# Row sums turned before the reciprocal instead of after it, in the attention stage of an attention and MLP kernel

## The chip, the cores and the metric

The kernel runs on one core of a Trainium2 chip. The metric is the device time in microseconds of one execution. Before the change it is 834.61 us, the median of 3 runs (834.24 to 835.53).

## The reference: attention, then two MLPs

Attention over 4 x 8 heads of 576 rows with 64 elements, with a decay bias from cumulative sums, and on its output (2304 tokens x 512) two MLPs. What the change touches is the division of the softmax by its sum:

```python
scores = np.where(causal, -1000000000.0, scores + np.minimum(bias, 0.0))
scores = scores - np.max(scores, axis=-1, keepdims=True)
attn = np.exp(scores)
attn = attn / (np.sum(attn, axis=-1, keepdims=True) + 1e-09)
return np.matmul(attn, v).astype(np.float32)
```

The first MLP computes (h - tanh(h)) @ w_out with h = x @ w_in (512 to 2048 to 512), the second a softmax-weighted, normalised hidden layer (512 to 1024 to 512). Their code is not touched.

## The kernel before, in words

Heads are worked in 16 pairs. A head's 576 rows are four tiles of 128 and a tail of 64; the tails of a pair's two heads share one tile, so a pair has 9 tiles (`TILES`). The attention stage is a software pipeline of slots, numbered -1 to 17: slot s loads and turns q and k of pair s+1, scores and exponentiates pair s, turns the probabilities of pair s-1 and multiplies them by V, and ends and scales pair s-2. Slots -1 to 3 and 14 to 17 are written out; slots 4 to 13 are a hardware loop of two slots a turn. "Slot 11" below is the one in which pair 11 is scored. In slots 16 and 17 no scores are left, and the first tiles of the first MLP's first chunk stand between the attention's matmuls.

There is no scheduler. Each engine has its own instruction list in the order of the code, and semaphores are the only ties between them; a wait stops everything behind it on its engine.

What each engine does for a slot:

- TensorE: `score` (three float32r products a tile, a mask matmul last), `turn_p` (transposes of the probabilities into PSUM, units A01, A2, A3, T, B01, B2, B3), `turn_qk` (transposes of q and k), `attend` (probabilities times V: `attend(-2, 1, ...)` ends the second head of pair s-2, `attend(-1, 0, ...)` does the first head of pair s-1) and, once a pair, the turn of the 9 columns with the softmax denominators (L1354 to L1360).
- VectorE: `bias` (L1000, adds the cumulative bias to the scores, PSUM to SBUF, and finds the row's extreme), `p_lo` (L983, the low part of the turned probabilities: PSUM minus the rounded high part), `x_add` and `x_low_part` (L1023, L1014, sums of the attend product), and `denominators` (L1025 to L1033).
- ACT: `p_hi` (L737, rounds the turned probabilities to the high part), `exp` (L746, with the row sum accumulated into a column of `row_sum`), `qk_copy` (L763), `x_low_part(0)` (L778), `rden_rows_copy` (L765 to L771).
- POOL: `sums` (L539, L542, copies the tail of the cumulative sums), `split_qk` (L557, L560), `scale_x` (L579, multiplies by the spread reciprocals), `split_v` (L592, L595).
- SP: the loads, the store of `rden_row` to HBM (L444, L446) and its broadcast back (L462).

The denominators of a pair are 9 columns of 128 values, one column a tile. VectorE adds 1e-9 (L1031) and takes the reciprocal (L1033) of the whole 128 x 9 array in SBUF; TensorE turns it into 9 rows of 128 in PSUM (L1360), ACT copies the rows to SBUF (L771), and SP stores them so that they can be read back broadcast over 64 partitions for `scale_x` in the next slot.

TensorE's first `attend(-1, 0, 0)` of a slot waits for `p_lo("T")`, which VectorE issues after `bias(0, 0)`, `bias(0, 1)`, `x_add(0)`, `p_lo("A01")`, `bias(1, 0)`, `bias(1, 1)`, `denominators()`, `p_lo("A2")`, `bias(0, 2)`, `bias(1, 2)`, `p_lo("A3")`, `x_low_part(1)` and `x_add(1)`. TensorE's `score(3)` waits for `bias(0, 2)`, whose PSUM it writes over.

Of the kernel before, what the change touches and what calls it, by code (L numbers as in the profile page):

```python
# [6 lines left out]
ALU = mybir.AluOpType  # L7
# [7 lines left out]
P = 128  # L15
# [35 lines left out]
def build_transformer(nc, q, k, v, s, w_in, w_out, w2_in, w2_out, g_ln, out):  # L51
# [59 lines left out]
    with ctx:  # L111
# [12 lines left out]
        with ExitStack() as phase:  # L124
            sb = tensors(phase, attention_words)
            qkT_hi = [sb(f"qkT_hi{n}", [P, QK_W], F32R) for n in range(2)]
            qkT_lo = [sb(f"qkT_lo{n}", [P, QK_W], F32R) for n in range(2)]
            probs = [sb(f"probs{n}", [P, PW]) for n in range(2)]
            pT_hi = sb("pT_hi", [P, 2, PT_W], F32R)

            v_parts = [sb(f"v_parts{n}", [P, NT, 4 * D], F32R) for n in range(2)]
            ident_b = sb("ident_b", [P, P], BF16)
            mask_b = sb("mask_b", [P, P], BF16)
            upper_b = sb("upper_b", [P, TAIL], BF16)
            lower_b = sb("lower_b", [P, TAIL], BF16)
            tail_mask_b = sb("tail_mask_b", [P, TAIL], BF16)
            neg_max = [sb(f"neg_max{n}", [P, TILES]) for n in range(2)]
            row_sum = [sb(f"row_sum{n}", [P, TILES]) for n in range(2)]
            den = [sb(f"den{n}", [P, TILES]) for n in range(2)]
            rden = [sb(f"rden{n}", [P, TILES]) for n in range(2)]  # L140
            rden_row = sb("rden_row", [TILES, P])

            w1i_words = GATE_W + FT * 2 * DM
            sb("gap", [P, w1i_words - sum(attention_words)])
            cum_bc = [sb(f"cum_bc{n}", [P, 2, S]) for n in range(2)]
            cum_tail = sb("cum_tail", [P, S])
            v_raw = [sb(f"v_raw{n}", [P, NT, 2 * D]) for n in range(2)]
            pT_lo = sb("pT_lo", [P, 2, PT_W], F32R)
            rden_T = [sb(f"rden_T{n}", [P, S]) for n in range(2)]
            qk_flat = [sb(f"qk_flat{n}", [P, FULL * P]) for n in range(2)]  # L150
            x_low = sb("x_low", [P, S])
            x_sum = sb("x_sum", [P, S])
# [64 lines left out]
        turn_ps = {"A01": bank(3), "A2": bank(4), "A3": bank(3), "T": bank(4), "B01": bank(3), "B2": bank(5), "B3": bank(4)}  # L217
        qk_ps = bank(5)

        rden_ps = bank(6)[0:TILES, 0:P]  # L220
        x_ps = psum[:, 7 * BANK - X_CUT:7 * BANK - X_CUT + S]
        h_ps = [bank(n, CH) for n in (0, 1, 2, 3)]
        y_ps = [bank(m, CH) for m in (4, 5, 6, 7)]
# [31 lines left out]
        biased = sem("biased")  # L255
        exped = sem("exped")
        den_step = sem("den_step")
        turned_rden = sem("turned_rden")
        rden_rows = sem("rden_rows")
        turned_p = sem("turned_p")  # L260
        p_hi_done = sem("p_hi_done")
# [407 lines left out]
        def _(act):  # L669
# [60 lines left out]
            def slot(sl):  # L730
                def p_hi(unit):

                    if sl.runs(-1):
                        pair, half, par = sl.pair(-1)
                        act.wait_ge(turned_p, UNITS * pair + NTH[unit])
                        for ps, to in pieces(unit):
                            hi = act.activation(to(pT_hi), ps, ACT.Copy)  # L737
                        hi.then_inc(p_hi_done, 1)

                def exp(h, t):  # L740

                    if sl.runs(0):
                        pair, half, par = sl.pair(0)
                        at, width, col = tile_at(h, t)
                        act.wait_ge(biased, TILES * pair + nth(sl, h, t)[0])
                        act.activation(probs[par][:, at:at + width], probs[par][:, at:at + width], ACT.Exp,  # L746
                                       bias=neg_max[par][:, col:col + 1], scale=-1.0,
                                       accum_out=row_sum[par][:, col:col + 1]).then_inc(exped, 1)

                def qk_copy(n):  # L750

                    if sl.runs(1):
                        pair, half, par = sl.pair(1)
                        at, width = QK_PART[n]
                        act.wait_ge(turned_qk, 3 * pair + n + 1)

                        if sl.fixed and sl.s <= 0:
                            to = qkT_hi[par][:, at:at + width]
                        else:
                            to = qk_flat[n % 2][:, 0:width]  # L760
                            if n != 1:
                                act.wait_ge(qk_lo, 3 * pair + (n == 2))
                        act.activation(to, qk_bank(sl, n)[:, 0:width], ACT.Copy).then_inc(qk_copied, 1)  # L763

                def rden_rows_copy():  # L765

                    if sl.runs(-1):
                        pair, half, par = sl.pair(-1)
                        act.wait_ge(turned_rden, pair + 1)
                        wait(act, rden_out, 32 * pair)  # L770
                        act.activation(rden_row[:, :], rden_ps, ACT.Copy).then_inc(rden_rows, 1)  # L771

                def x_low_part(h):

                    if sl.runs(-2):
                        pair, half, par = sl.pair(-2)
                        act.wait_ge(attended, 2 * pair + h + 1)
                        act.activation(x_low[h * D:(h + 1) * D, :], x_ps[(1 - h) * D:(2 - h) * D, :],  # L778
                                       ACT.Copy).then_inc(x_low_done, 1)

                if sl.fixed and sl.s == 0:
                    for h in range(2):
                        exp(h, 0)
                        exp(h, 1)
                    qk_copy(0)
                    exp(0, 2)
                    qk_copy(1)
                    exp(1, 2)
                    qk_copy(2)
                    exp(0, 3)  # L790
                    exp(1, 3)
                    exp(None, FULL)
                    return
                x_low_part(0)
                p_hi("A01")
                exp(0, 0)
                p_hi("A2")
                qk_copy(0)
                exp(0, 1)
                exp(1, 0)  # L800
                exp(1, 1)
                first_w1i(sl, 0)
                p_hi("A3")
                qk_copy(1)
                rden_rows_copy()
                exp(0, 2)
                if sl.fixed and sl.s == LAST:

                    act.wait_ge(turned_p, UNITS * PAIRS)
                    act.wait_ge(v_split, 2 * PAIRS)  # L810
                    step(0, 0)
                p_hi("T")
                first_w1i(sl, 1)
                qk_copy(2)
                exp(1, 2)
                p_hi("B01")
                exp(0, 3)
                first_w1i(sl, 2)
                p_hi("B2")
                exp(1, 3)  # L820
                first_w1i(sl, 3)
                p_hi("B3")
                exp(None, FULL)
# [82 lines left out]
        def _(dve):  # L906
# [69 lines left out]
            def slot(sl):  # L976
# [29 lines left out]
                def x_low_part(h):  # L1006

                    if sl.runs(-2):
                        pair, half, par = sl.pair(-2)
                        dve.wait_ge(attended, 2 * pair + h + 1)  # L1010
                        if h == 1 and sl.runs(-1):

                            dve.wait_ge(rden_rows, pair + 2)
                        dve.tensor_copy(x_low[h * D:(h + 1) * D, :], x_ps[(1 - h) * D:(2 - h) * D, :]).then_inc(x_low_done, 1)  # L1014

                def x_add(h):
# [8 lines left out]
                def denominators():  # L1025

                    if sl.runs(-1):
                        pair, half, par = sl.pair(-1)
                        dve.wait_ge(exped, TILES * (pair + 1))
                        wait(dve, turned_rden, pair - 1)  # L1030
                        dve.tensor_scalar(den[par][:, :], row_sum[par][:, :], 1e-9, None, ALU.add).then_inc(den_step, 1)  # L1031
                        dve.wait_ge(den_step, 2 * pair + 1)
                        dve.reciprocal(rden[par][:, :], den[par][:, :]).then_inc(den_step, 1)  # L1033

                def qk_rest(n):

# [28 lines left out]
                p_lo("A01")  # L1065
                bias(1, 0)
                bias(1, 1)
                denominators()
                p_lo("A2")
                bias(0, 2)  # L1070
                bias(1, 2)
                first_w1i(sl, 0)
# [110 lines left out]
        def _(pe):  # L1183
# [58 lines left out]
            def slot(sl):  # L1242
# [108 lines left out]
                            mm = pe.transpose(to[:, TAIL:TAIL + P], q_raw[par][:, FULL, :], ident[:, :])  # L1351
                        mm.then_inc(turned_qk, 1)

                def turn_rden():  # L1354

                    if sl.runs(-1):
                        pair, half, par = sl.pair(-1)
                        pe.wait_ge(den_step, 2 * (pair + 1))
                        wait(pe, rden_rows, pair)
                        pe.transpose(rden_ps, rden[par][:, :], ident[:, :]).then_inc(turned_rden, 1)  # L1360

                if sl.fixed and sl.s == 0:
                    score(0, 1)
# [10 lines left out]
                turn_qk(0)  # L1374
                score(2)
                attend(-2, 1, 0)
                turn_p("A3")
                turn_qk(1)
                turn_rden()
                attend(-2, 1, 1, 2, 3, 4)  # L1380
                turn_p("T")
                turn_qk(2)
# [109 lines left out]
```

## Time and profile before

| | |
|---|---|
| median of 3 runs | 834.61 us |
| profiled execution, in all | 835.15 us |
| its span | 833.3 us |
| TensorE matmuls busy | 816.6 us, 98% |
| VectorE busy | 446.4 us, 54% |
| ACT busy | 384.7 us, 46% |
| POOL busy | 200.2 us, 24% |
| mean granted TensorE clock | 0.996 |

```profile
## 2 busy tenths in 40 slices
PE   6999999998999999999999999999999999999998
DVE  5789999998854332233223322334647554455442
ACT  4899899888543322223223222324524333333322
POOL 3687787788100000000000000000022211221110
PEclk9899999999999999999999999999999999999999
```

PE is TensorE, DVE is VectorE. Each digit is the busy share of a fortieth of the span, 20.8 us, in tenths. The attention stage is the first ten or eleven slices: there VectorE and ACT are as busy as TensorE, and POOL nearly so; behind it TensorE is alone. A matmul's end is modelled, so a busy TensorE is not one at its peak. In the rows, times are microseconds unless marked ns; in brackets stands the idle time of an engine before an instruction and what ended it.

### The profile page before, as it was taken

The page shows a single profiled execution, that of the slowest core. Times are in us where ns is not written, and L with a number is a line of the kernel's source. Part 1 is how long each engine was busy: PE and PEld are TensorE (multiplying, and loading weights), DVE is VectorE, ACT ScalarE, POOL GpSimd, SP SyncE. Part 2 cuts the span into 40 slices and gives each one's busy share as a digit, 9 for nine tenths or more (in the row PEclk, how much of TensorE's full clock was granted, in tenths as well). Part 3 has the DMA queues.
Part 4 walks back from the last instruction along what each step waited for, and adds up shares of the span by engine and source line. Part 5 has one row for each costly group of instructions (what it writes and reads, how often), then busy time and mean ns, then how long its engine had stood idle before and what let it go on. Part 6 is the DMA issues. An engine that isn't in the chain of part 4 may idle for free.

```text
span 833.3 us, 14383 instructions
## 1 busy us (share of the span) xinstructions
PE 816.6 (98%) x4552; PEld 706.7 (85%) x4552; DVE 446.4 (54%) x1029; ACT 384.7 (46%) x868; POOL 200.2 (24%) x242
## 2 busy tenths in 40 slices
PE   6999999998999999999999999999999999999998
PEld 5888888887888888888888888999988888888886
DVE  5789999998854332233223322334647554455442
ACT  4899899888543322223223222324524333333322
POOL 3687787788100000000000000000022211221110
PEclk9899999999999999999999999999999999999999
DMA  7464565454433100000000000000200000000001
GB/s 180 127 167 121 150 163 150 123 140 145 139 118 112 51 1 0 1 1 0 0 0 0 0 0 0 0 1 26 76 0 9 31 13 25 25 25 13 25 25 39
DMA packets 77715, 46.30 MB, mean 56 GB/s; under 512 B 59824, under 2 KB 68144, under 8 KB 77680
## 3 DMA queue, kind: packets, MB, share of 16 engines
q1 hardware_dynamic: 75232, 45.19, 18.9%
q10 hardware_dynamic: 2448, 0.66, 0.4%
q8 instruction: 19, 0.31, 0.2%
q14 instruction: 16, 0.13, 0.1%
HBM read 40.97 MB, written 4.87 MB: 55 GB/s over the span
## 4 chain that ended last, share of the span: by engine, by line
PE 89%; DVE 3%; SPq 2%; issue 2%; DMA 2%; ACT 0%; DVEq 0%; ACTq 0%
PE psum L1201 24%; PE psum L1214 24%; PE psum L1416 12%; PE psum L1444 11%; PE psum L1299 6%; PE psum L1256 4%; PE psum L1332 3%; PE psum L1430 2%; PE psum L1348 1%; PE psum L1274 1%; PE psum L1260 1%; SPq L390 1%; DVE pT_lo L983 1%; DMA stage<-in_k 1%; DVE probs L1000 1%
## 5 line engine op out<-in xcount | busy, mean ns | idle before, releaser
L1201 PE MATMUL psum<-x_hi,w1i 128*128 128x464 f32 (+1 forms) x640 | 185.7, 371 | 0.5 <-DVE w1i L933 0.5
L1214 PE MATMUL psum<-gate_hi,w1o 128*128 128x464 f32 (+1 forms) x640 | 146.5, 371 | 0.0
L1201 PEld LDWEIGHTS psum<-x_hi,w1i 128*128 128x128 f32 x640 | 119.8, 188 | 14.9 <-DVE w1i L933 0.9
L1214 PEld LDWEIGHTS psum<-gate_hi,w1o 128*128 128x128 f32 x640 | 120.2, 188 | 13.6
L967 DVE TENSOR_TENSOR gate_lo<-gate,gate_hi 128x464 fp32r<-128x464 f32 (+1 forms) x80 | 51.1, 639 | 135.6 <-ACT gate_hi L721 135.6
L1201 PE MATMUL psum<-x_lo,w1i 128*128 128x464 f32 (+1 forms) x320 | 118.8, 371 | 0.0
L721 ACT ACTIVATE gate_hi<-gate 128x464 fp32r<-128x464 f32 (+1 forms) x80 | 47.1, 589 | 146.9 <-PE psum L1214 137.6
L635 POOL CAST y_hi<-xT 128x512 fp32r (+1 forms) x18 | 11.0, 612 | 387.6 <-PE psum L1201 384.2
L957 DVE TENSOR_TENSOR gate<-psum,gate 128x464 f32<-128x464 f32 (+1 forms) x80 | 51.0, 637 | 97.2 <-ACT gate L710 97.1
L710 ACT ACTIVATE gate<-psum 128x464 f32<-128x464 f32 (+1 forms) x80 | 44.1, 551 | 107.2 <-PE psum L1201 105.2
L1444 PE MATMUL psum<-w2o,lnT_hi 128*128 128x512 f32 x288 | 91.9, 400 | 0.6 <-DVE lnT_lo L1157 0.6
L746 ACT ACTIVATE probs<-probs,neg_max 128x128 f32<-128x128 f32 (+2 forms) x144 | 84.0, 584 | 11.1 <-DVE neg_max L1000 9.5
L1214 PE MATMUL psum<-gate_lo,w1o 128*128 128x464 f32 (+1 forms) x320 | 80.0, 371 | 0.0
L1416 PE MATMUL psum<-w2i,y_hi 128*128 128x512 f32 x288 | 77.4, 390 | 0.0
L983 DVE TENSOR_TENSOR pT_lo<-psum,pT_hi 128x512 fp32r<-128x512 f32 (+3 forms) x160 | 73.0, 480 | 8.0 <-ACT pT_hi L737 7.0
L737 ACT ACTIVATE pT_hi<-psum 128x512 fp32r<-128x512 f32 (+3 forms) x160 | 63.9, 433 | 17.9 <-PE psum L1332 17.4
L1000 DVE CUSTOM_DVE_ANT_0 probs<-psum,cum_bc 128x128 f32<-128x128 f32 (+3 forms) x128 | 58.6, 483 | 16.0 <-PE psum L1260 11.7
L1201 PEld LDWEIGHTS psum<-x_lo,w1i 128*128 128x128 f32 x320 | 60.1, 188 | 6.7
L1214 PEld LDWEIGHTS psum<-gate_lo,w1o 128*128 128x128 f32 x320 | 60.1, 188 | 6.5
L1416 PEld LDWEIGHTS psum<-w2i,y_hi 128*128 128x128 f32 x288 | 54.0, 188 | 11.8 <-issue 0.2
L1444 PEld LDWEIGHTS psum<-w2o,lnT_hi 128*128 128x128 f32 x288 | 52.9, 189 | 12.0 <-issue 1.0
L1332 PE MATMUL psum<-ident,probs 128*128 128x128 f32 x400 | 59.6, 280 | 0.5 <-ACT probs L746 0.5
(115 smaller groups left out, 1272.3 us busy)
## 6 DMA issues: line engine op xcount, KB each, us to landing
cum_bc<-cum_dram SPq DMA_DIRECT2D x16, 576.0 KB, 4.8
rden_T<-rden_dram SPq DMA_DIRECT2D x32, 144.0 KB, 3.0
out_x<-out_sb SPq DMA_DIRECT2D x18, 256.0 KB, 2.0
stage<-in_q SPq DMA_DIRECT2D x32, 128.0 KB, 2.5
v_raw<-in_v SPq DMA_DIRECT2D x32, 128.0 KB, 3.7
stage<-in_moe_w_in SPq DMA_DIRECT2D x16, 256.0 KB, 3.1
stage<-in_moe_w_out SPq DMA_DIRECT2D x16, 256.0 KB, 3.4
stage<-in_k SPq DMA_DIRECT2D x28, 128.0 KB, 2.3
```

What stands on the lines that cost most here:

```text
L737: hi = act.activation(to(pT_hi), ps, ACT.Copy)
L746: act.activation(probs[par][:, at:at + width], probs[par][:, at:at + width], ACT.Exp, bias=neg_max[par][:, col:col + 1], scale=-1.0, accum ...
L957: dve.tensor_tensor(gate[j % 2][:, 0:n], h_ps[j % 4][:, 0:n], gate[j % 2][:, 0:n], ALU.subtract).then_inc(gate_done, 1)
L967: dve.tensor_tensor(gate_lo[j % 2][:, 0:n], gate[j % 2][:, 0:n], gate_hi[j % 2][:, 0:n].bitcast(F32), ALU.subtract).then_inc(gate_lo_done, 1)
L983: lo = dve.tensor_tensor(to(pT_lo), ps, to(pT_hi).bitcast(F32), ALU.subtract)
L1000: dve.tensor_tensor_reduce(probs[par][:, at:at + width], tail_bank(sl) if h is None else score_ps[h][t], cum_tail[:, :] if h is None else ...
L1201: mm = pe.matmul(h_ps[j % 4][:, 0:wide(c)], wp[j][:, kt, :], xp[:, kt, 0:wide(c)], start=(n == 0), stop=(n == 3 * KT - 1))
L1214: mm = pe.matmul(y_ps[m][:, 0:wide(c)], wp[j][:, m * P:(m + 1) * P], gp[j % 2][:, 0:wide(c)], start=(j == 0 and wp is w1o_hi and gp is gat ...
L1299: mm = pe.matmul(x_ps[:, c0:c1], v_parts[par][:, j, 2 * h * D:2 * h * D + P], pp[:, h, j * STEP + c0:j * STEP + c1], start=(j == 0 and n = ...
L1332: mm = pe.transpose(ps[:, n * P:(n + 1) * P], probs[par][:, at:at + P], ident[:, :])
L1416: mm = pe.matmul(h2_ps[par][:, half * BANK:(half + 1) * BANK], yp[par][:, kt, :], wp[kt][:, 4 * half:4 * half + 4, :].rearrange("q f p -> ...
L1444: mm = pe.matmul(out_ps[par], lp[par][:, f, :], wp[f][:, :], start=(f == 0 and n == 0), stop=(f == FT2 - 1 and n == 2))
```

## The change

The row sums are turned as they are, and the addition and the reciprocal are done on the turned rows, in PSUM: `turn_sums` on TensorE turns `row_sum` into 9 rows of 128 in PSUM bank 6; VectorE adds 1e-9 from there into another part of the bank and takes the reciprocal of that straight into `rden_row` in SBUF. ACT's copy, the arrays `den` and `rden`, and VectorE's wait on `rden_rows` ahead of `x_low_part(1)` are gone. Two calls move: `denominators()` on VectorE from before `p_lo("A2")` to behind it, and the turn on TensorE from behind `turn_qk(1)` to before `turn_p("A3")`.

```diff
@@ PSUM @@
-        rden_ps = bank(6)[0:TILES, 0:P]
+        sum_ps = bank(6)[0:TILES, 0:P]
+        den_ps = bank(6)[0:TILES, P:2 * P]
@@ ACT @@
-                def rden_rows_copy():
-
-                    if sl.runs(-1):
-                        pair, half, par = sl.pair(-1)
-                        act.wait_ge(turned_rden, pair + 1)
-                        wait(act, rden_out, 32 * pair)
-                        act.activation(rden_row[:, :], rden_ps, ACT.Copy).then_inc(rden_rows, 1)
...
                 qk_copy(1)
-                rden_rows_copy()
                 exp(0, 2)
@@ VectorE @@
                         dve.wait_ge(attended, 2 * pair + h + 1)
-                        if h == 1 and sl.runs(-1):
-
-                            dve.wait_ge(rden_rows, pair + 2)
...
-                        dve.wait_ge(exped, TILES * (pair + 1))
-                        wait(dve, turned_rden, pair - 1)
-                        dve.tensor_scalar(den[par][:, :], row_sum[par][:, :], 1e-9, None, ALU.add).then_inc(den_step, 1)
-                        dve.wait_ge(den_step, 2 * pair + 1)
-                        dve.reciprocal(rden[par][:, :], den[par][:, :]).then_inc(den_step, 1)
+                        dve.wait_ge(turned_sum, pair + 1)
+                        dve.tensor_scalar(den_ps, sum_ps, 1e-9, None, ALU.add).then_inc(den_step, 1)
+                        dve.wait_ge(den_step, pair + 1)
+                        wait(dve, rden_out, 32 * pair)
+                        dve.reciprocal(rden_row[:, :], den_ps).then_inc(rden_rows, 1)
...
                 bias(1, 1)
+                p_lo("A2")
                 denominators()
-                p_lo("A2")
                 bias(0, 2)
@@ TensorE @@
-                def turn_rden():
+                def turn_sums():
...
-                        pe.wait_ge(den_step, 2 * (pair + 1))
+                        pe.wait_ge(exped, TILES * (pair + 1))
                         wait(pe, rden_rows, pair)
-                        pe.transpose(rden_ps, rden[par][:, :], ident[:, :]).then_inc(turned_rden, 1)
+                        pe.transpose(sum_ps, row_sum[par][:, :], ident[:, :]).then_inc(turned_sum, 1)
...
                 attend(-2, 1, 0)
+                turn_sums()
                 turn_p("A3")
                 turn_qk(1)
-                turn_rden()
                 attend(-2, 1, 1, 2, 3, 4)
```

VectorE in the middle of a loop slot, before; L1031 and L1033 are the denominators, the L983 behind them is `p_lo("A2")` and the last L1000 is `bias(0, 2)`:

```order
L1000 ISA probs,neg_max<-psum,cum_bc 128x256 [waits scored]
L1000 ISA neg_max 128x1
L1031 TENSOR_SCALAR den<-row_sum 128x9 [waits turned_rden,exped]
L1033 RECIPROCAL rden<-den 128x9 [waits den_step]
L983 TENSOR_TENSOR pT_lo<-psum,pT_hi 128x3x128 [waits p_hi_done]
L1000 ISA probs,neg_max<-psum,cum_bc 128x384 [waits scored]
```

The same place after; L991 is `bias`, L974 `p_lo`, L1018 and L1021 the denominators:

```order
L991 ISA probs,neg_max<-psum,cum_bc 128x256 [waits scored]
L991 ISA neg_max 128x1
L974 TENSOR_TENSOR pT_lo<-psum,pT_hi 128x3x128 [waits p_hi_done]
L1018 TENSOR_SCALAR psum<-psum 9x128 [waits turned_sum]
L1021 RECIPROCAL rden_row<-psum 9x128 [waits rden_out,den_step]
L991 ISA probs,neg_max<-psum,cum_bc 128x384 [waits scored]
```

The two operations stand one `p_lo` later, have 9 partitions of 128 elements instead of 128 of 9, and the first waits for TensorE.

TensorE in the same stretch, before; L1299 is `attend`, L1332 `turn_p("A3")`, L1348 `turn_qk(1)`, L1360 the turn of the reciprocals:

```order
L1299 MATMUL psum<-pT_hi,v_parts 128x128 [waits p_lo_done,x_added]
L1299 MATMUL psum<-pT_hi,v_parts 128x448
L1299 MATMUL psum<-pT_lo,v_parts 128x128
L1299 MATMUL psum<-pT_lo,v_parts 128x448
L1332 MATMUL psum<-ident,probs 128x128 [waits p_lo_done,exped]
L1332 MATMUL psum<-ident,probs 128x128 x3
L1348 MATMUL psum<-ident,stage 128x128 [waits qk_copied]
L1348 MATMUL psum<-ident,stage 128x128 x3
L1360 MATMUL psum<-ident,rden 9x128 [waits rden_rows,den_step]
```

And after; L1287 is `attend`, L1348 now the turn of the sums, L1320 `turn_p("A3")`, L1336 `turn_qk(1)`:

```order
L1287 MATMUL psum<-pT_hi,v_parts 128x128 [waits p_lo_done,x_added]
L1287 MATMUL psum<-pT_hi,v_parts 128x448
L1287 MATMUL psum<-pT_lo,v_parts 128x128
L1287 MATMUL psum<-pT_lo,v_parts 128x448
L1348 MATMUL psum<-ident,row_sum 9x128 [waits rden_rows,exped]
L1320 MATMUL psum<-ident,probs 128x128 [waits p_lo_done,exped]
L1320 MATMUL psum<-ident,probs 128x128 x3
L1336 MATMUL psum<-ident,stage 128x128 [waits qk_copied]
L1336 MATMUL psum<-ident,stage 128x128 x3
```

The turn has moved ahead of eight transposes and waits for ACT's exps instead of VectorE's reciprocal.

## Rows read from the trace of the kernel before

**Rows 1.** Windows of slots 4 and 11: busy per engine (PE, PEld, DVE, ACT, POOL), clock

```profile
55.51:67.34 11.83, 11.79 (x100) 10.22 (x100) 10.79 (x33) 10.91 (x34) 9.27 (x12) 1.00 0.52 134
140.89:153.18 12.29, 12.12 (x100) 10.18 (x99) 11.25 (x33) 11.06 (x35) 9.78 (x12) 1.00 0.57 145
```

**Rows 2.** Chain of waits in slot 11: start, duration, what

```profile
149.19 0.70 DVE pT_lo L983
...
149.93 0.90 PE psum L1299 x4
```

**Rows 3.** Timeline of VectorE, slot 11: start, duration, instruction

```profile
142.37 0.29 DVE L1000 CUSTOM_DVE_ANT_0 probs<-psum,cum_bc 128x128 f32<-128x128 f32 x1 [0.71 <-PE psum L1260]
...
144.70 0.63 DVE L1031 TENSOR_SCALAR den<-row_sum 128x9 f32<-128x9 f32 x1
...
145.49 0.53 DVE L983 TENSOR_TENSOR pT_lo<-psum,pT_hi 128x384 fp32r<-128x384 f32 x1
```

**Rows 4.** Timeline of POOL, slot 11

```profile
144.65 0.66 POOL L539 COPY cum_tail<-cum_bc 64x576 f32<-64x576 f32 x1 [0.17 <-POOL v_parts L595]
```

**Rows 5.** Timeline of VectorE, slot 4

```profile
59.32 0.16 DVE L1031 TENSOR_SCALAR den<-row_sum 128x9 f32<-128x9 f32 x1
59.52 0.22 DVE L1033 RECIPROCAL rden<-den 128x9 f32<-128x9 f32 x1
59.65 0.53 DVE L983 TENSOR_TENSOR pT_lo<-psum,pT_hi 128x384 fp32r<-128x384 f32 x1
```

**Rows 6.** Single lines: count, ns shortest/median/longest, first and last start

```profile
L1031 DVE TENSOR_SCALAR den<-row_sum x16: 158/613/639, 21.9 to 204.9; 128x9 f32<-128x9 f32 x16
...
L1033 DVE RECIPROCAL rden<-den x16: 215/216/216, 22.1 to 205.2; 128x9 f32<-128x9 f32 x16
...
L1134 DVE RECIPROCAL small<-small x18: 143/146/147, 625.1 to 816.0; 128x1 f32<-128x1 f32 x18
...
L1142 DVE TENSOR_SCALAR small<-small x18: 153/154/156, 625.9 to 816.9; 128x1 f32<-128x1 f32 x18
```

**Rows 7.** Timeline of VectorE, the additions of slots 5, 6 and 14

```profile
71.14 0.43 DVE L1031 TENSOR_SCALAR den<-row_sum 128x9 f32<-128x9 f32 x1
...
83.24 0.63 DVE L1031 TENSOR_SCALAR den<-row_sum 128x9 f32<-128x9 f32 x1
...
181.70 0.61 DVE L1031 TENSOR_SCALAR den<-row_sum 128x9 f32<-128x9 f32 x1
```

**Rows 8.** Groups by shape, 60 to 174 us: busy us, mean ns, idle

```profile
L1014 DVE COPY x_low<-psum 64x576 f32<-64x576 f32 x10 | 7.5, 751 | 0.3
...
L1000 DVE CUSTOM_DVE_ANT_0 probs<-psum,cum_bc 128x128 f32<-128x128 f32 x18 | 5.1, 283 | 6.2 <-PE psum L1260 6.2
```

**Rows 9.** Timeline of TensorE, slot 11

```profile
144.30 0.48 PE L1299 MATMUL psum<-pT_lo,v_parts 128*128 128x128 f32 x2
...
147.84 0.49 PE L1256 MATMUL psum<-qkT_hi 64*128 64x512 f32 x2
```

**Rows 10.** The line of the turn

```profile
L1360 PE MATMUL psum<-ident,rden x16: 272/278/422, 25.1 to 205.6; 128*9 128x128 f32 x16
```

**Rows 11.** Timeline of POOL, slot 11

```profile
150.60 1.29 POOL L560 TENSOR_TENSOR qkT_lo<-qk_flat,qkT_hi 128x512 fp32r<-128x512 f32 x1 [0.18 <-POOL qkT_hi L557]
152.53 1.43 POOL L579 TENSOR_TENSOR xT<-x_sum,rden_T 128x576 f32 x1 [0.64 <-POOL qkT_lo L560]
```

**Rows 12.** Timeline, slots 1 and 2

```profile
23.74 0.56 DVE L1000 CUSTOM_DVE_ANT_0 probs<-psum,cum_bc 128x384 f32<-128x384 f32 x1 [1.03 <-PE psum L1260]
...
39.52 0.69 DVE L983 TENSOR_TENSOR pT_lo<-psum,pT_hi 128x512 fp32r<-128x512 f32 x1
...
40.35 0.55 PE L1299 MATMUL psum<-pT_hi,v_parts 128*128 128x128 f32 x2
```

**Rows 13.** Timeline of VectorE, slot 16

```profile
209.38 1.63 DVE L933 TENSOR_TENSOR w1i<-stage,w1i 128x512 fp32r<-128x512 f32 x1
```

**Rows 14.** Timeline of TensorE's weight loads, slot 11

```profile
149.93 0.30 PEld L1299 LDWEIGHTS psum<-pT_hi,v_parts 128*128 128x128 f32 x2 [0.38 <-DVE pT_lo L983]
```

More of the change, by code:

```diff
@@ L138, in build_transformer @@
             row_sum = [sb(f"row_sum{n}", [P, TILES]) for n in range(2)]
-            den = [sb(f"den{n}", [P, TILES]) for n in range(2)]
-            rden = [sb(f"rden{n}", [P, TILES]) for n in range(2)]
             rden_row = sb("rden_row", [TILES, P])
@@ L257, in build_transformer @@
         den_step = sem("den_step")
-        turned_rden = sem("turned_rden")
+        turned_sum = sem("turned_sum")
         rden_rows = sem("rden_rows")
```

## The prediction

> **What bounds the kernel now.** I read the views in this order. The page's first part, shown in the table above, says that TensorE is busy for nearly the whole span, which would make every edit on VectorE free. But the change touches only the attention stage, so I looked at one of its steps ("slots", 12.3 us each) with the window view: TensorE 12.12, VectorE 11.25, ACT 11.06, POOL 9.78 of 12.29 us [rows 1]. All four engines are near the slot's length, so the order of work, not a busy share, decides.
>
> Both windows there run from one first score matmul of TensorE to the next: slot 4 takes 11.83 us, slot 11, in the loop, 12.29. Two things need explaining: what ties the engines together, and where the extra 0.46 us comes from.
>
> The chain of waits names the tie [rows 2]: TensorE stands before the first attend matmuls until VectorE's p_lo("T") is done. Followed backwards through VectorE's own timeline [rows 3], p_lo("T") at 149.19 [rows 2] closes a row of instructions without a gap that began with bias(0, 0) at 142.37, which had itself waited 0.71 us for TensorE's scores. So a slot is one round trip: TensorE from its start to the scores' end and over to VectorE, 142.37 - 140.89 = 1.48 us; VectorE to the end of p_lo("T"), 149.19 + 0.70 - 142.37 = 7.52; 0.04 to TensorE's start at 149.93; TensorE to the next slot, 153.18 - 149.93 = 3.25. The sum is 12.29, the measured slot. Whatever VectorE gains or loses between bias(0, 0) and p_lo("T") is gained or lost by the slot, and `denominators()` stands exactly there.
>
> The 0.46 us are in that stretch too. In the loop the addition of 1e-9 takes 0.63 us, from 144.70 to 145.33 [rows 3]; POOL's cum_tail copy runs from 144.65 to 145.31 [rows 4]. In slot 4 the same instruction takes 0.16 us [rows 5]. It sits until POOL's copy is done: of 16 instances the shortest is 158 ns and the median 613 [rows 6].
> The Trainium skill (SBUF — State Buffer, "Who interferes with whom") states that a `tensor_scalar` in a 2-port mode takes an exclusive pair of ports that it shares with GpSimd; the trace agrees, with an end 0.02 us behind POOL's.
> Of 16 pairs, nine (slots 6 to 14, from 83.24 to 181.70) show 0.61 to 0.64 us, slot 5 0.43 [rows 7], slot 16 about half as much as they, the other five 0.16 or 0.17.
>
> **The change, part by part.**
> Removed from VectorE per pair: the block from the addition's start to p_lo("A2"). In a loop slot that is 145.49 - 144.70 = 0.79 us [rows 3]; where POOL is out of the way, 59.65 - 59.32 = 0.33 us [rows 5].
>
> Added on VectorE: the same two operations, but on 9 partitions x 128 elements instead of 128 partitions x 9. An engine with lanes by partition pays for the elements in a row, so this is 14 times the length.
> - The addition, PSUM to PSUM: the copy x_low, 576 elements from PSUM, takes 751 ns, and the 128-element bias from PSUM 283 ns [rows 8]. The slope between them is 468/448 = 1.04 ns for an element. I take 0.28 us. It has no operand in SBUF, so I charge no hold by POOL. Bounds 0.16 (the old one alone) and 0.63 (the old one held).
> - The step to the reciprocal behind its semaphore: 59.52 - 59.48 = 0.04 us [rows 5].
> - The reciprocal, PSUM to SBUF. The trace has no long one, but two short ones: 216 ns for 9 elements and 146 ns for 1 [rows 6]. An ordinary small operation goes from 153 (1 element) to 158 ns (9) [rows 6]. So the 70 ns are the reciprocal's own, 70/8 = 8.75 ns for an element. For 128: 146 + 127 x 8.75 = 1257 ns. The low bound lets the elements beyond the ninth pass at the 1.04 ns of other operations: 216 + 119 x 1.04 = 340 ns. The high bound adds the fixed 0.15 us of a small operation once more, for the PSUM source: 1.40. I take 1.26, the straight line through the two reciprocal rows, since no ordinary operation shows such a step between 1 and 9.
> - The next instruction starts 59.74 - 59.65 = 0.09 us before a reciprocal's end [rows 5].
> The new block is 0.28 + 0.04 + 1.26 - 0.09 = 1.49 us.
> The Trainium skill (Vector Engine (DVE) Microarchitecture Reference, "5.2 Measured stream behaviour on trn2") has built-in one-source operations at 1.04 ns a column; by that the reciprocal would be 0.34 us, which is the first rival below. The Trainium skill's page VectorE: DVE Perf Modes ("First, the fixed hardware budget") gives the reciprocal an iterated divide with a repeat count of 8; 8 x 1.04 = 8.3 ns an element is an estimate from these pages, the block would be 1.43 us by it, and the two reciprocal rows side with it.
>
> Its place: `denominators()` moves behind p_lo("A2"). Both stand inside the gap-free stretch, so the move changes nothing in the sum. It does make VectorE wait for TensorE's turn. p_lo("A2") would start at about 144.76 and end at 145.29 (0.53 long); TensorE reaches the turn behind attend(-2, 1, 0), whose last matmuls run from 144.30 for 0.48 us, and a turn lasts 0.28 [rows 9, 10], so the sums lie in PSUM at 144.78 + 0.28 = 145.06. Margin 0.2 us: no wait. The sums come from the exps of the slot before, which ACT ends before it takes up this slot's work, so TensorE doesn't wait for ACT there.
>
> Removed from ACT: one small copy a pair. The round trip doesn't run through it: 0. Removed on TensorE: a short wait before the old turn, which only moves idle time ahead of the wait for p_lo("T"): 0. VectorE's wait on rden_rows before x_low goes; it was met already. SP's store of rden_row stands behind loads in its queue and is wanted a slot later: 0. The bias(0, 2) behind the block ends 0.7 us later, near 147.2, before TensorE's score(3) at 147.84 that reuses its bank [rows 9]: covered by 0.6 us.
>
> **The sum.**
> - Slots 6 to 14, nine: 1.49 - 0.79 = 0.70 each, 6.3 us. There POOL's own round is about 12.3 us a slot: 9.78 busy [rows 1] and the gaps between twelve instructions, the longest the 0.64 us before xT, and all its gaps follow its own instructions [rows 11]. The new slot of 13.0 us is longer than that, so POOL doesn't bind.
> - Slot 5: the old block is 0.79 - 0.63 + 0.43 = 0.59; +0.90.
> - Slots 2 to 4 and 15: 1.49 - 0.33 = 1.16 each. In slot 2 TensorE starts 0.14 us after p_lo("T") ends (39.52 + 0.69 to 40.35) [rows 12] where 0.04 is the bare step, so 0.1 is slack; slot 3 is alike. Sum 4 x 1.16 - 0.2 = 4.4.
> - Slot 1: VectorE idles 1.03 us before bias(0, 2) [rows 12] and more later; 0.
> - Slot 16: no scores, TensorE fills its waits with the first MLP chunk. But the delay pushes VectorE's w1i part (already held by POOL, 1.63 us) [rows 13] past the matmuls that want it: 0 to 1.0, I take 0.4.
> Total 6.3 + 0.9 + 4.4 + 0.4 = 12.0 us. The MLP stages are untouched. Against the profiled execution (833.3 us of span, 835.15 in all, so 1.85 around it) this is 847.1; that execution was 0.5 above the median of 834.61, so the forecast is 834.6 + 12.0 = 846.6 us.
>
> **Rivals.** What a measurement can tell from no change is about 0.2%, 1.7 us.
> A. *The reciprocal streams like any other operation* (0.34 us, block 0.28 + 0.04 + 0.34 - 0.09 = 0.57). Its place is the same stretch; it decides from a reciprocal under 0.79 - 0.28 - 0.04 + 0.09 = 0.56 us on. Loop slots would gain 0.22 each, but POOL's 12.3 us would stop them once VectorE stops being held: the slack is about 1.2 us in all (POOL's qk split ends at 151.9, TensorE wants it at 153.2 [rows 1, 11]). The four unheld slots lose 4 x 0.24 - 0.2 and slot 5 0. Together -1.2 + 0.8 = -0.4: 834.2 us, not slower. For it: no long reciprocal is in the trace. Against it: the 70 ns between 1 and 9 elements.
> B. *TensorE's wait for p_lo("T") isn't the whole of the round trip*, and its idle time (0.38 us before its weight load [rows 14]) absorbs part of the delay: 0.70 - 0.38 = 0.32 in nine slots, 0.8 in the others: 2.9 + 0.5 + 3.2 = 6.6: 841.2. Against it: the sum of 12.29 closes, with 0.04 us between the engines.
> C. *The new handoff opens a wait too*: the turn comes too late or PSUM costs more, 0.2 us in each of 14 slots: +2.8 more, 849.4. The margin above is only 0.2 us.
>
> **Chances.** Forecast 0.74, A 0.05, B 0.08, C 0.13. The range: a reciprocal of 1.20 takes 0.06 x 14 = 0.8 off and slot 16 another 0.4, 845.4; one of 1.40 with slot 16 at 1.0 gives 849.2. I take in most of C and part of the way to B: 843.5 to 850.0. Slower by over 0.2%: the forecast, B and C, 0.95, less a little for cases unseen: 0.94; A gives within 0.2% 0.04 and faster 0.02.
>
> **What would show it.** A reciprocal row of 9x128 near 1.26 us (0.34 says A). No addition held to 0.6 us any more. Loop slots of 13.0 us between score starts, with POOL's waits now named after other engines, TensorE's wait for p_lo("T") near 1.1 us a slot. If the slots lengthen by much less than the block, B is right; if VectorE idles before the addition, C. I would be wrong altogether if the granted clock, 1.00 in these slots [rows 1], fell with TensorE's longer pauses.

## The result and the profile after

The changed kernel takes 842.94 us (median of 6 runs, 842.21 to 844.09), the kernel before 835.07 (6 runs, 834.21 to 837.54): a ratio of 1.0091, with a 95% interval of 1.0076 to 1.0107. It is slower, as forecast, but by 7.9 us and not by 12.0; 842.94 lies 0.6 us under the low end of the range. The profiled execution (span 842.3, in all 844.09) is the longest of the six.

The new instructions of the line view (count, ns shortest/median/longest) answer to [rows 6]:

```profile
L1018 DVE TENSOR_SCALAR psum<-psum x16: 276/277/287, 24.3 to 214.1; 9x128 f32<-9x128 f32 x16
...
L1021 DVE RECIPROCAL rden_row<-psum x16: 945/946/947, 24.6 to 214.4; 9x128 f32<-9x128 f32 x16
```

The addition takes 0.28 us as forecast, and none is held any more. The reciprocal takes 0.946 us, four times the old one's 0.216, where the prediction had 1.257.

Two slots in the window view (busy per engine, clock), to lay beside [rows 1]:

```profile
57.78:70.52 12.74, 11.96 (x101) 10.16 (x100) 11.61 (x33) 10.88 (x34) 9.34 (x12) 1.00 0.54 141
146.94:159.65 12.71, 11.95 (x100) 10.15 (x100) 11.60 (x33) 10.85 (x34) 9.73 (x12) 1.00 0.52 140
```

Slots 4 and 11, 11.83 and 12.29 us before, now take the same 12.7: the difference between the slots with and without POOL's hold is gone. The clock is still 1.00. VectorE's timeline of slot 11, against [rows 3]:

```profile
148.41 0.29 DVE L991 CUSTOM_DVE_ANT_0 probs<-psum,cum_bc 128x128 f32<-128x128 f32 x1 [0.70 <-PE psum L1248]
...
150.74 0.55 DVE L974 TENSOR_TENSOR pT_lo<-psum,pT_hi 128x384 fp32r<-128x384 f32 x1
151.21 0.28 DVE L1018 TENSOR_SCALAR psum<-psum 9x128 f32<-9x128 f32 x1
151.61 0.95 DVE L1021 RECIPROCAL rden_row<-psum 9x128 f32<-9x128 f32 x1
152.49 0.48 DVE L991 CUSTOM_DVE_ANT_0 probs<-psum,cum_bc 128x384 f32<-128x384 f32 x1
...
155.67 0.69 DVE L974 TENSOR_TENSOR pT_lo<-psum,pT_hi 128x512 fp32r<-128x512 f32 x1
```

The new block is 152.49 - 151.21 = 1.28 us (forecast 1.49), the stretch from bias(0, 0) to the end of p_lo("T") 156.36 - 148.41 = 7.95 us (7.52 before). TensorE waits at its far end, 0.38 us in [rows 14], 0.97 now:

```profile
156.42 0.30 PEld L1287 LDWEIGHTS psum<-pT_hi,v_parts 128*128 128x128 f32 x2 [0.97 <-DVE pT_lo L974]
```

TensorE's turn of the sums ran from 150.67 for 0.27 us, done at 150.94, 0.27 before VectorE's addition: the handoff opens no wait.

Slot lengths by TensorE's first score matmul of each slot (slots 6 to 14 from the start of 6 to that of 15; slot 15 up to the first `turn_p` of slot 16, at 202.07 and 210.63 us; slot 16 from there to the first down matmul of the MLP, at 222.16 and 231.05):

| | before | after | difference | forecast |
|---|---|---|---|---|
| slot 1 | 13.41 | 13.52 | +0.11 | 0 |
| slots 2 to 4 and 15 | 11.96, 11.94, 11.83, 11.87 | 12.79, 12.80, 12.74, 12.70 | +3.43 | +4.4 |
| slot 5 | 12.09 | 12.73 | +0.64 | +0.9 |
| slots 6 to 14 | 110.77 | 114.68 | +3.91 | +6.3 |
| slot 16 | 20.09 | 20.42 | +0.33 | +0.4 |
| sum | | | +8.4 | +12.0 |

Slot 1 began 0.47 us later in this execution, and the rest of the kernel after the first down matmul takes 611.14 us before and 611.25 after; with the 8.4 that makes the 9.0 between the two spans. The medians are 7.9 apart.

### The profile page after: what moved, and what is told of

It is laid out like the page before. It is cut to its first block, busy times and chain, and to the rows that moved or that the text cites. A ratio compares the mean times of both kernels' runs of the same rounds, so it can differ in the third digit from the quotient of the medians.

```text
span 842.3 us, 14323 instructions
## 1 busy us (share of the span) xinstructions
PE 816.2 (97%) x4552; PEld 706.4 (84%) x4552; DVE 454.8 (54%) x1029; ACT 382.7 (45%) x852; POOL 199.8 (24%) x242
## 4 chain that ended last, share of the span: by engine, by line
PE 82%; DVE 10%; issue 5%; DMA 2%; DVEq 1%; ACT 1%; SPq 0%; ACTq 0%
PE psum L1189 24%; PE psum L1202 24%; PE psum L1404 12%; PE psum L1432 11%; PE psum L1287 4%; DVE pT_lo L974 4%; DVE probs L991 2%; PE psum L1244 2%; PE psum L1418 2%; PE psum L1320 1%; PE psum L1262 1%; DVE x_low L1002 1%; PE psum L1248 1%; DVE x_sum L1011 1%; DMA cum_bc<-cum_dram 1%
## 5 line engine op out<-in xcount | busy, mean ns | idle before, releaser
L1202 PEld LDWEIGHTS psum<-gate_hi,w1o 128*128 128x128 f32 x640 | 120.1, 188 | 13.6
L974 DVE TENSOR_TENSOR pT_lo<-psum,pT_hi 128x512 fp32r<-128x512 f32 (+3 forms) x160 | 73.1, 482 | 6.1 <-ACT pT_hi L737 5.6
L1287 PE MATMUL psum<-pT_hi,v_parts 128*128 128x128 f32 (+2 forms) x192 | 56.1, 331 | 11.8 <-DVE pT_lo L974 10.9
L991 DVE CUSTOM_DVE_ANT_0 probs<-psum,cum_bc 128x128 f32<-128x128 f32 (+3 forms) x128 | 57.6, 474 | 15.7 <-PE psum L1248 11.0
```

The lines of the kernel that those rows point to most:

```text
L974: lo = dve.tensor_tensor(to(pT_lo), ps, to(pT_hi).bitcast(F32), ALU.subtract)
L991: dve.tensor_tensor_reduce(probs[par][:, at:at + width], tail_bank(sl) if h is None else score_ps[h][t], cum_tail[:, :] if h is None else ...
L1202: mm = pe.matmul(y_ps[m][:, 0:wide(c)], wp[j][:, m * P:(m + 1) * P], gp[j % 2][:, 0:wide(c)], start=(j == 0 and wp is w1o_hi and gp is gat ...
L1287: mm = pe.matmul(x_ps[:, c0:c1], v_parts[par][:, j, 2 * h * D:2 * h * D + P], pp[:, h, j * STEP + c0:j * STEP + c1], start=(j == 0 and n = ...
```

## Experiments

Theory R: the whole price is the reciprocal's length, and VectorE's delay goes one to one into the slot. Theory P: POOL's own round of 12.3 us is the second bound in the loop. Ratios are to the kernel before, in runs on the same chip (its median there 833.9 to 835.1 us).

**The reciprocal replaced by a multiplication** (e1)

```diff
-dve.reciprocal(rden_row[:, :], den_ps).then_inc(rden_rows, 1)
+dve.tensor_scalar(rden_row[:, :], den_ps, 1.0, None, ALU.mult).then_inc(rden_rows, 1)
```

> The changed kernel with its reciprocal (0.95 us) replaced by a multiplication by 1.0 of the same shape; the output lacks the division. Theory R (the reciprocal's length is the price, and VectorE's delay goes one to one into the slot): the multiplication takes 0.28 us, the block 0.28 + 0.12 + 0.28 - 0.07 = 0.6 us; slots 2 to 4 and 15 fall from 12.75 to about 12.1, loop slots to POOL's round of 12.3; the time falls by 0.66 x 4 + 0.45 x 10 = 7 us, to 834.5 to 836. Theory H (the handoff from TensorE, the PSUM operands or TensorE's moved turn cost a good part): it stays over 838.

Measured: 835.73 us, ratio 1.0013 (1.0000 to 1.0027). Timeline of VectorE and a window of one loop slot:

```profile
146.13 0.28 DVE L1018 TENSOR_SCALAR psum<-psum 9x128 f32<-9x128 f32 x1
146.54 0.28 DVE L1021 TENSOR_SCALAR rden_row<-psum 9x128 f32<-9x128 f32 x1
146.81 0.56 DVE L991 CUSTOM_DVE_ANT_0 probs<-psum,cum_bc 128x384 f32<-128x384 f32 x1
```

```profile
141.86:154.06 12.20, 11.96 (x100) 10.16 (x99) 11.07 (x33) 10.97 (x34) 9.69 (x12) 1.00 0.60 146
```

0.67 us less of one instruction takes 0.51 us from the slot of 12.71; the block's successor took 0.08 us longer again (0.56 against 0.48), and its start was no longer drawn forward by 0.07. All but about 1 us of the change's 7.9 is the reciprocal (by the interval, all but 0 to 2.3). The 1 us is a net figure: slots 2 to 4 take 12.2 us, 0.2 to 0.4 more than before, the loop slots 12.2, 0.1 less. That they come out below P's 12.3 doesn't speak against P: POOL's own round in this kernel is still 12.3 us (from 128.71 to 141.02, each idle time in it ended by its own instruction), and its lead over TensorE isn't used up yet. H falls: the handoff, the PSUM operands and the moved turn are still in this kernel.

**Half of the reciprocal** (e2)

```diff
+pool.memset(rden_row[:, :], 1.0)
...
-dve.reciprocal(rden_row[:, :], den_ps).then_inc(rden_rows, 1)
+dve.reciprocal(rden_row[:, 0:P // 2], den_ps[:, 0:P // 2]).then_inc(rden_rows, 1)
```

> The changed kernel with the reciprocal of the first 64 of 128 elements alone; the other half of the rows is left at 1. Theory R with a price per element: by the line through 216 ns (9 elements) and 946 ns (128), 6.1 ns each, it takes 0.55 us; the slot falls by 0.39 from 12.74 to 12.35, the time by 13 x 0.39 = 5 us to about 838. If the reciprocal in this form has a large fixed part (PSUM source, 9 partitions) instead, it stays at 0.8 us or more and the time over 840.5.

Measured: 836.75 us, ratio 1.0030 (1.0019 to 1.0041). The line and the window of a loop slot:

```profile
L1022 DVE RECIPROCAL rden_row<-psum x16: 544/545/547, 24.0 to 207.5; 9x64 f32<-9x64 f32 x16
```

```profile
142.06:154.36 12.30, 11.95 (x100) 10.15 (x99) 11.19 (x33) 10.98 (x34) 9.77 (x11) 1.00 0.57 143
```

0.545 us, as the price per element says, and a slot 0.41 us shorter for 0.40 us less reciprocal: one to one. Each set against its own runs of the kernel before, the ratios of 1.0091 and 1.0030 are 5.1 us apart, as expected.

**The price per element** (e4): in the kernel before, at the end of VectorE's work

```diff
+for parts in (P, TILES):
+    for n in (1, 5, 9, 16, 32, 64, 128, 256):
+        for src in (act2[0], ln_ps[0]):
+            dve.reciprocal(act2[1][0:parts, 0:n], src[0:parts, 0:n]).then_inc(probs_const, 1)
...
```

> The kernel before with reciprocals of 1, 5, 9, 16, 32, 64, 128 and 256 elements added at the end of VectorE's work, each from SBUF and from PSUM, on 128 and on 9 partitions, and additions of 1, 9, 128 and 256. Theory L (a price per element from the first on): straight lines with one slope of 6 to 9 ns an element; the 128 of the changed kernel at 0.95 us says 6.1. Rival S: a steeper piece up to some 9 elements (8.75 ns between 1 and 9) and a flatter one behind it, or a slope that differs between SBUF and PSUM. Theory L would put 256 from PSUM at 1.73 us.

Measured, timeline of VectorE (`act` is in SBUF):

```profile
824.20 0.16 DVE L1191 RECIPROCAL act<-act 128x1 f32<-128x1 f32 x1
...
825.05 0.21 DVE L1191 RECIPROCAL act<-act 128x9 f32<-128x9 f32 x1
...
826.13 0.35 DVE L1191 RECIPROCAL act<-act 128x32 f32<-128x32 f32 x1
...
828.09 0.95 DVE L1191 RECIPROCAL act<-act 128x128 f32<-128x128 f32 x1
829.08 0.96 DVE L1191 RECIPROCAL act<-psum 128x128 f32<-128x128 f32 x1
830.07 1.75 DVE L1191 RECIPROCAL act<-act 128x256 f32<-128x256 f32 x1
...
838.37 0.94 DVE L1191 RECIPROCAL act<-psum 9x128 f32<-9x128 f32 x1
...
841.12 1.75 DVE L1191 RECIPROCAL act<-psum 9x256 f32<-9x256 f32 x1
...
843.69 0.23 DVE L1196 TENSOR_SCALAR act<-act 128x128 f32<-128x128 f32 x1
843.95 0.29 DVE L1196 TENSOR_SCALAR act<-psum 128x128 f32<-128x128 f32 x1
```

One line: (1.75 - 0.95)/128 = 6.25 ns an element at the long end, (0.21 - 0.16)/8 = 6.3 at the short one, 0.01 us between SBUF and PSUM, and 0.02 us or less between 128 and 9 partitions. Theory L holds, S falls. An addition of 128 elements costs 0.23 us from SBUF and 0.29 from PSUM.

**The addition left out** (e3), in the kernel before

```diff
-dve.tensor_scalar(den[par][:, :], row_sum[par][:, :], 1e-9, None, ALU.add).then_inc(den_step, 1)
-dve.wait_ge(den_step, 2 * pair + 1)
-dve.reciprocal(rden[par][:, :], den[par][:, :]).then_inc(den_step, 1)
+dve.reciprocal(rden[par][:, :], row_sum[par][:, :]).then_inc(den_step, 1)
...
-pe.wait_ge(den_step, 2 * (pair + 1))
+pe.wait_ge(den_step, pair + 1)
```

> The kernel before with the addition of 1e-9 left out and nothing else (the sums are 1 or more, so float32 doesn't show it). Theory P (POOL's own round of 12.3 us is the second bound in the loop): VectorE's block falls from 0.79 to 0.17 us, but loop slots stay at 12.3 once POOL's lead of 1.2 us is used up; the time falls by 1 to 2 us, to 833 to 834. Rival N (only the round trip TensorE to VectorE and back binds): all loop slots fall to 11.8, by 0.5 x 10 = 5 us, to 830.

Measured: 835.88 us, ratio 1.0013 (1.0000 to 1.0025): no gain at all. But the slots do what P says. The window of a loop slot, and TensorE at its start:

```profile
137.96:150.25 12.29, 12.01 (x100) 10.19 (x101) 10.57 (x32) 10.83 (x35) 9.77 (x11) 1.00 0.55 145
```

```profile
137.96 0.33 PE L1254 MATMUL psum<-qkT_hi 64*128 64x128 f32 x2 [0.17 <-POOL qkT_lo L560]
```

Slots 2 to 6 take 11.7 to 12.0 us; from the slot at 101.13 on TensorE waits for POOL's split and they take 12.3. From the start of slot 2 to that of slot 15 it is 157.3 us against 158.6: 1.3 won. In the profiled execution more than that was lost behind it, where it takes 645.0 us against 643.1. Windows of 2 us in that kernel:

```profile
202.00:204.00 2.00, 2.00 (x10) 1.85 (x10) 1.94 (x4) 0.54 (x2) 2.00 (x2) 0.58 0.54 208
204.00:206.00 2.00, 2.00 (x13) 1.96 (x11) 1.04 (x2) 0.20 (x2) 1.54 (x2) 0.57 0.01 2
```

and of the kernel before, at the same place:

```profile
204.00:206.00 2.00, 1.53 (x11) 1.48 (x12) 1.97 (x7) 1.26 (x4) 1.92 (x3) 1.00 0.94 360
```

After a stretch from 200 to 202 us in which TensorE was busy 0.70 of 2.00 us, most of the next 4 us ran at the lower of its two clock levels (a granted clock near 0.5, 1.2 GHz). Nine of its 10 runs have a mean clock of 0.992 to 0.996, the kernel before mostly 0.997 to 1.000.

**VectorE's move alone** (e5), in the kernel before

```diff
-                denominators()
                 p_lo("A2")
+                denominators()
```

> The kernel before with one of the change's moves alone: VectorE's denominators() behind p_lo("A2"), with the old shapes and the old place of TensorE's turn. Theory R: both stand in the gap-free stretch, so the move itself is free; the addition then starts near 145.3 of slot 11, when POOL's first copy is just over, and POOL's round of 12.3 us still sets the loop. TensorE waits 0.1 to 0.3 us more for the reciprocal, ahead of a wait that it has anyway: 833 to 835.5, no change. Rival M (the move is a part of the change's price, because bias(0, 2), TensorE's score(3) or the turn come late): slots of 12.4 to 12.6 us and 836 or more.

Measured: 838.47 us, ratio 1.0050 (1.0031 to 1.0070). Both are half wrong: the slots are nearly R's (12.28 us in the loop; 0.7 us more in all from slot 2 to slot 15, most of it in slots 2 to 5, and no run shows from what), the time is M's. The rest comes behind the start of slot 15. In slot 16, on VectorE and TensorE:

```profile
206.10 1.12 DVE L1031 TENSOR_SCALAR den<-row_sum 128x9 f32<-128x9 f32 x1
```

```profile
207.52 0.38 PE L1360 MATMUL psum<-ident,rden 128*9 128x128 f32 x1 [0.95 <-DVE rden L1033]
```

```profile
208.00:210.00 2.00, 2.00 (x10) 1.92 (x10) 0.69 (x3) 0.21 (x1) 0.00 (x0) 0.50 0.01 2
```

The addition now meets a longer POOL instruction (L605, 1.19 us), takes 1.12 us where it took 0.34, TensorE waits 0.95 for the reciprocal, and from 208 to 210 us it has the lower clock. From the start of slot 15 to the end it is 645.9 us against 643.1. In the changed kernel this doesn't happen: none of its 16 additions takes more than 0.287 us, and TensorE waits for no reciprocal there.

**POOL's copies replaced by DMAs**, in the kernel before (e6) and in the changed one (e7); POOL's waits on cum_copied go with the copies

```diff
+wait(sp, biased, TILES * pair)
...
+for h in range(2):
+    sp.dma_start(cum_tail[h * TAIL:(h + 1) * TAIL, :],
+                 cum_dram[bass.ds(2 * pair + h, 1), :].to_broadcast([TAIL, S])).then_inc(tail_in[par], 16)
...
-pool.tensor_copy(cum_tail[0:TAIL, :], cum_bc[par][0:TAIL, 0, :]).then_inc(cum_copied, 1)
...
-pool.tensor_copy(cum_tail[TAIL:P, :], cum_bc[par][TAIL:P, 1, :]).then_inc(cum_copied, 1)
```

> The kernel before, with cum_tail filled by two broadcast DMAs from SP a slot instead of two POOL copies; the arithmetic is the same. Theory P (in the loop POOL's round of 12.3 us and its hold of VectorE's addition cost 0.46 us a slot): POOL's round falls to 12.3 - 1.65 = 10.6 us, nothing holds the addition, all slots take 11.8 us; 10 loop slots and slot 14 gain 0.45 each: 5 us less, 829 to 830; if TensorE's clock is granted at half speed for a stretch near slot 16 as in the kernel without the addition, 2 us less of the gain, 831 to 832. Rival D: SP's queue (about 9 us of issues a slot) gets too long and loads come late: loop slots of 12.3 us or more, 834 and up.

> The changed kernel with the same two DMAs in place of POOL's copies. If VectorE's round trip with the 0.95 us reciprocal is the only bound after the change (theory R), freeing POOL changes nothing: slots of 12.73 us, 842 to 843. If POOL holds or delays anything there as well, the slots fall under 12.6 and the time under 841.

Measured: e6 844.98 us, ratio 1.0119 (1.0097 to 1.0141); e7 846.10, ratio 1.0137 (1.0117 to 1.0158). Windows of two loop slots of e6:

```profile
108.35:121.52 13.17, 11.84 (x102) 10.15 (x101) 10.97 (x34) 11.00 (x34) 8.39 (x10) 1.00 0.58 157
150.19:162.01 11.82, 11.79 (x100) 10.23 (x100) 10.83 (x34) 10.94 (x34) 8.45 (x10) 1.00 0.58 162
```

and what TensorE waited for from 60 to 120 us (total, times, longest):

```profile
PE psum L1337 <- DMA stage<-in_k: 4.4, 5, 1.3
```

D is right about the time: SP's queue goes round in 12.7 to 12.8 us a slot, from cum_bc to cum_bc, no wait of it is recorded there, and k comes late. P is right where SP is not late: two slots, behind one of 15.73 us that let SP catch up, take 11.82 and 11.89, and in the first POOL has time to idle:

```profile
155.94 0.61 POOL L548 CAST qkT_hi<-qk_flat 128x512 fp32r<-128x512 f32 x1 [1.23 <-ACT qk_flat L750]
```

In e7 the undisturbed loop slots stay at 12.73 us with POOL busy 8.78:

```profile
122.09:134.82 12.73, 11.99 (x100) 10.15 (x99) 11.60 (x33) 10.87 (x34) 8.78 (x10) 1.00 0.69 154
```

So after the change POOL isn't a bound, as R says; its total of 846 is a miss of mine, made of 1.5 us at the start and single slots of up to 13.6; in the two longest TensorE waited 0.8 and 0.9 us for k, as in e6.

**One DMA for both heads** (e8), an attempt at a kernel that beats both

```diff
+def spread(dram, pair):
+    return dram[bass.ds(2 * pair, 2), :].rearrange("h (o s) -> h o s", o=1).to_broadcast([2, D, S])
...
+sp.dma_start(cum_tail[:, :], spread(cum_dram, pair)).then_inc(tail_in[par], 16)
...
+sp.dma_start(rden_T[par][:, :], spread(rden_dram, pair)).then_inc(rden_in[par], 16)
```

> The kernel before, with cum_tail filled by one broadcast DMA for both heads instead of two POOL copies, and the spread reciprocals also loaded by one DMA instead of two. In the kernel with two cum_tail DMAs, SP issued for 12.9 us a slot and the loop slots took 12.9, but a slot in which SP wasn't late took 11.82. If one DMA for both heads costs SP 0.55 us as a single one does, SP's round is 12.9 - 1.1 = 11.8 us and the slots fall to 11.8 to 11.9 us: 4 to 5 us less than before, 829 to 831; with a stretch of half clock more near slot 16, up to 2 us of it are lost. If the issue time goes by rows and not by DMA, SP's round stays at 12.3 to 12.9 us and the time at 834 or more.

Measured: 957.35 us, ratio 1.1464 (1.1447 to 1.1482). The issue takes 0.58 us as hoped, but what lies behind it stalls; SP's queue, and VectorE waiting for cum_tail:

```profile
101.64 0.58 SPq L442 DMA_DIRECT2D cum_tail<-cum_dram  x1
102.49 7.39 SPq L391 DMA_DIRECT2D v_raw<-in_v  x2
```

```profile
95.30 0.76 DVE L987 CUSTOM_DVE_ANT_0 probs<-psum,cum_tail 128x576 f32<-128x576 f32 x1 [4.61 <-DMA cum_tail<-cum_dram]
```

Neither theory had that. In e6 the same two v_raw issues take 0.94 us. The loop slots take 20.5 to 21.4 us, the mean granted clock is 0.921, and the DMA engines are not busy meanwhile (the last two figures are their mean busy share and GB/s):

```profile
90.00:92.00 2.00, 1.83 (x15) 1.60 (x13) 0.69 (x3) 1.59 (x4) 1.32 (x2) 1.00 0.13 52
105.00:107.00 2.00, 2.00 (x10) 1.88 (x9) 0.69 (x1) 1.12 (x3) 0.00 (x0) 0.50 0.13 48
```

Two of 16 engines at work would be a share of 0.125. Of the 200 half-microseconds from 60 to 160 us, 49 have a share of 0.11 to 0.14, against 4 in e6. The Trainium skill (DMA: Bandwidth & Descriptors, "Why a DMA increments its semaphore by 16 and not by 1") states that the number of DMA engines used must divide the slowest dimension, which is 2 in the merged source. The shares agree with that, but no run varies the shape alone, so the cause isn't isolated. No version tried beats the kernel before.

## Why the prediction was wrong

- *The step that failed is the size of the reciprocal.* "146 + 127 x 8.75 = 1257 ns" should have been 946 ns. The two rows were 8 elements apart and from different places: 146 ns for one element in the second MLP, 216 ns for nine in the attention. Measured side by side, one element takes about 0.16 us and nine 0.21 [e4], so each row was up to 0.01 us off (why isn't shown), and a slope over 8 elements carries that 16 times over when it is stretched to 128. The 0.31 us too much, in 14 slots, come to 4.3 us, about the 4.1 us by which the forecast of 12.0 exceeded the measured 7.9. The smaller misses nearly cancel (the terms below). The range took 1.20 as the lowest likely value, though the same rows, read with 0.02 us of doubt at one end, allow 6.25 ns.
- *That it isn't a streaming operation was right.* Rival A's 0.34 us is a third of what was measured. The repeat count of 8 that the Trainium skill states (VectorE: DVE Perf Modes, "First, the fixed hardware budget") was a poor second witness. The page gives no time per element; 8 x 1.04 = 8.3 ns was my estimate from it. Measured are 6.25 ns, which is six cycles of 1.04 ns. The measurement decides, and I had taken the agreement of two wrong numbers, 8.3 and 8.75, for a confirmation.
- *The round trip is confirmed, one to one.* Reciprocals of 0.55 and 0.95 us give slots of 12.30 and 12.71 us (e2, after). Rival B falls. Rival C falls too: VectorE never idled before the addition, except for 1.4 us in slot 1, where TensorE ran at its lower clock level and its turn was late; slot 1 grew by 0.11 us only.
- *The hold by POOL is confirmed.* No addition is held in the changed kernel, and with POOL's copies gone (e6) the old addition takes a median of 161 ns instead of 613. But it wasn't the whole cause of the extra 0.46 us: with the addition left out (e3) the later loop slots still take 12.3.
- *POOL as the second bound is confirmed* by TensorE's new wait for it in e3 and by the slots of 11.82 and 11.89 us in e6, in which POOL idles.
- *The terms now.* Of the new block, the addition was right (0.28); the step to the reciprocal takes 0.12 us in the loop instead of 0.04, but 214.40 - 214.08 - 0.29 = 0.03 in slot 16, which is written out; the start of the next instruction lies 0.07 before the reciprocal's end (0.09). The bias(0, 2) behind it is 0.07 shorter, which no term had. In the loop 1.28 - 0.79 - 0.07 = 0.42 us a slot; slots 6 to 14 grew by 0.43 each, against 0.70 forecast.
- *That the move is free* holds in the loop of this change, where block and bias account for 0.42 of 0.43 us. Alone, in e5, the move costs 4 us by the medians; in the profile 2.8 of its 3.5 come behind the start of slot 15, and 0.7 in slots 2 to 14. I had not looked at what the addition would meet in slot 16.

## What to carry to other kernels

Turning data from many partitions with few elements into few partitions with many makes a VectorE instruction pay for the long side: a turn saved an ACT copy that nobody waited for and made a reciprocal of 0.22 us one of 0.95 on the path. A slope from two small instructions is no basis for one 14 times as long: give it the width that 0.01 to 0.02 us at either end make, or bound it from both sides and keep the middle open. Where two engines run for the same round, a hold of one by the other can be the symptom of the slower one's round, and freeing the held one gives only the slower one's lead (1.3 us in e3) until that round is shortened.

## What the runs showed of the hardware

- A reciprocal costs 6.25 ns an element from 1 to 256 elements, in SBUF and PSUM alike, with about 0.15 us besides.
- Single stretches of TensorE at its lower clock level are worth about 2 us of this kernel. In the profile of the kernel before, most of slot 1 ran at the lower level:

```profile
20.00:22.00 2.00, 1.54 (x8) 0.81 (x6) 1.58 (x10) 1.31 (x5) 0.46 (x1) 0.50 0.82 295
```

  It took 13.41 us; in e3, whose clock was 1.00 there (and 0.65 from 10 to 14 us instead), it took 11.08. An edit that makes slots shorter by 1 us can thus show as nothing, or as a loss. The stretches in e3 and e5 came behind idle time of TensorE, but in the changed kernel it is busy for only 0.65 of the 2 us from 206 to 208 us and the clock stays at 1.00. The pauses themselves weren't varied, so what brings a stretch on stays open.
- The custom bias instruction behind the long reciprocal takes 0.48 us instead of 0.55. Why stays open.
